# Zeroing the experts' sums on another engine, a new order of the first units' splits, and stores spread between loads

## Chip, cores and metric

The kernel runs on one core of one Trainium2 chip. The metric is the device time of one execution in microseconds; lower is better.

## Reference

Three layers follow each other, all in fp32.

```
attention: state = f[t]*state + outer(k[t], v[t]);  y[t] = q[t] @ state       B=4, H=8, S=768, D=48
gelu layer: h = x @ w_in;  g = h * sigmoid(1.702*h);  x2 = g @ w_out           x: 3072 x 384, FF=2048
experts:    p = probs / (sum(probs) + 1e-9)
            out = sum over e of p[:, e] * (relu(x2 @ w1[e]) @ w2[e])           E=4, w1[e]: 384 x 1024
```

## The kernel before

Every fp32 matrix product is made of three passes with operands split into a high part (fp32r, a copy made by ACT) and a low part (raw minus high, a subtraction by POOL or DVE): high by high, high by low, low by high.

**First part** (to about 660 us). Tokens are taken in 8 halves of 384. While the attention of half n+1 runs, the gelu layer of half n runs beside it, in slots: `hidden` for block `slot`, `layer_out` for block `slot - 2`. The last half (`moe(n)` on each engine, L850 for POOL, 16 blocks, 18 slots) has no attention beside it, so the engines prepare the first data of the experts there: weights of groups 0 and 1 and the tokens.

**Second part, the experts.** The 4 experts with 4 groups of 256 hidden columns each give 16 groups. Tokens come in three pairs of 1024 (`pr`). A unit is one group on one pair; 48 units: units 0 to 31 go over pairs 0 and 1 (groups 0 and 1 on pair 0, then on pair 1, then groups 2 and 3, ...), units 32 to 47 take pair 2 through all groups, with the weights loaded a second time (weight loads 16 to 31). On PE unit u is `first_layer(u)`, 33 matmuls of 512 columns with sums of blocks in place of a fourth of the products, and `second_layer(u)`, 48 matmuls of 384. The program order is first layer of unit 0, then for each u the first layer of u and the second layer of u-1. So units 0 and 1 have their first layers back to back.

What each engine does for unit u:

- ACT: `copy_x(u, 0..2)` (L1098) copies the bank `sum_x` to SBUF after the 1st, 2nd and 3rd stage of the first layer; `relu(u, 0..3)` (L1092) makes h_h.
- DVE: `sum_of(u, 1..5)` (L1410) adds banks and copies; `h_low(u, 0..3)` (L1416) makes h_l; `accumulate(u-1, 0..7)` (L1426) adds the second layer's result times the share to `acc`, the experts' sums (24 tiles of 128 tokens x 384, 8 a pair).
- PE's `first_layer(u)` waits in its middle for `hl_ready`, all four `h_low` of unit u-1, and for `x_copied`, the copies of unit u. PE's `second_layer` waits for the accumulations, since y has three banks.

`acc` lies in memory that earlier steps use, so it is set to zero late: by DVE in its loop over units, for pair 0 in unit 0 (L1442), for pairs 1 and 2 in units 2 and 4 (L1447), 3072 elements per partition each, always between the sums and the `h_low` and `accumulate` of that unit.

Preparing weights w: SP loads `we_raw` (L553) and `w_raw` (L558, named w2_raw in the code); POOL makes four sums of blocks (`weight_sums`, L801 to L809), ACT the high parts (`w1_high` L1064, `w2_high` L1072), POOL the low parts (`w1_low` L816, `w2_low` L827). Each of SP's loads waits until the low parts of the weights before are made. Preparing half-pair i of the tokens: SP loads `x_raw` (L567, x2_raw in the code, 2 DMAs) when the low parts of half-pair i-1 are made; sums of blocks (DVE L1355 to L1362 for i = 0 to 2, POOL L834 to L841 for i = 3), three high parts (`x_high`, ACT L1084), three low parts (`x_low`, DVE L1368 or POOL L847). Unit 0 needs half-pairs 0 and 1, unit 2 needs half-pairs 2 and 3.

All engines run their programs in order, and SP issues the DMAs in order: one queue, in which a wait holds up all that follows. ACT holds a fixed place for each split:

```
if u == 0:
    w2_high(1)
    for part in range(len(X_PARTS)):
        x_high(3, part)
```

stands behind unit 0's `relu`s and ahead of unit 1's `copy_x`. SP stores pairs 0 and 1 with two DMAs of 1536 KB (L591) between weight loads 18 and 19, once unit 31 is accumulated; pair 2 goes out tile by tile at the end (L598).

## Time and profile before

| | |
|---|---|
| median of 3 runs | 1444.72 us (1442.06 to 1447.53) |
| the profiled execution, its own time | 1443.81 us |
| its span, first to last instruction | 1442.1 us |
| PE busy in the span | 1397.3 us (97%) |
| DVE, POOL, ACT busy | 909.0, 633.6, 568.0 us |
| DMA share of its 16 engines | 23.4% |

The span is what the profiler saw between the first and the last instruction of this one execution; the execution's own time has 1.7 us around it. "Busy" adds up instructions and says nothing of which wait sets the end. PE is busy nearly all the time, so what can be gained without removing matmuls is at most the time in which PE waits, or runs at the lower clock. The lines of the rows below read: start in us from the span's start, duration, engine, line of the kernel, operation, output and input with their shapes, and in brackets how long the engine had stood idle before and who ended it. "x3" are three instructions in a row, and the duration is then that of all of them.

### The profile page before, as it was taken

To read this page: it belongs to the slowest core of one execution; us is meant where nothing else is said; L and a number is where in the kernel's file an instruction comes from. 1 tells how busy PE (TensorE), PEld (TensorE's weight loads), DVE (VectorE), ACT (ScalarE), POOL (GpSimd) and SP (SyncE) were. 2 spreads that over 40 slices of the span, in tenths; PEclk is the share of its full clock that TensorE was granted. 3 is DMA by queue.
4 is the path that set the end of the run, shared out by engine and by line. 5 is a ranking of instruction groups with operands and counts; after the bars stand their busy time and mean duration, and the time that the engine had idled before them with its cause. 6 is when DMAs were issued, how large, how long until landed. Compare 5 with 4: busy or idle time off the path is not lost.

```text
span 1442.1 us, 20967 instructions
## 1 busy us (share of the span) xinstructions
PE 1397.3 (97%) x8092; PEld 1315.9 (91%) x8092; DVE 909.0 (63%) x1375; ACT 568.0 (39%) x975; POOL 633.6 (44%) x711
## 2 busy tenths in 40 slices
PE   6889999999999999998999999999999999999999
PEld 5789999999999999996889999999999998999998
DVE  7785747565566656355666666666666666666666
ACT  5563534344444435244232233233223433343331
POOL 8785656556564737356122121222212363444430
PEclk9999999999999999999999999999999999999999
DMA  8534242332425150022010110101010113111111
GB/s 141 116 103 72 63 61 75 46 90 37 100 28 108 18 108 14 26 69 93 11 34 12 34 33 11 34 22 34 11 34 29 60 33 132 54 56 45 44 56 45
DMA packets 239700, 79.00 MB, mean 55 GB/s; under 512 B 188656, under 2 KB 238064, under 8 KB 239600
## 3 DMA queue, kind: packets, MB, share of 16 engines
q1 hardware_dynamic: 239600, 77.66, 23.4%
q8 instruction: 64, 1.05, 0.3%
q14 instruction: 36, 0.29, 0.1%
HBM read 67.83 MB, written 9.78 MB: 54 GB/s over the span
## 4 chain that ended last, share of the span: by engine, by line
PE 84%; POOL 5%; DVE 3%; ACT 3%; issue 2%; DMA 2%; SPq 0%; ACTq 0%; DVEq 0%; POOLq 0%
PE bank L1730 9%; PE bank L1732 9%; PE bank L1731 9%; PE bank L1679 8%; PE bank L1680 8%; PE bank L1681 8%; PE bank L1551 5%; PE bank L1643 4%; PE bank L1644 4%; PE bank L1645 4%; PE bank L1479 4%; PE bank L1477 4%; PE bank L1478 4%; PE bank L1590 2%; POOL g_l L779 2%
## 5 line engine op out<-in xcount | busy, mean ns | idle before, releaser
L1426 DVE SCALAR_TENSOR_TENSOR acc<-bank,p_n,acc 128x384 f32<-128x384 f32 x384 | 235.0, 613 | 67.5 <-PE bank L1732 63.0
L779 POOL TENSOR_TENSOR g_l<-sig,g_h 128x384 fp32r<-128x384 f32 x128 | 169.9, 1328 | 235.6 <-ACT g_h L1000 235.6
L1730 PE MATMUL bank<-w_h,h_h 128*128 128x384 f32 x768 | 258.2, 336 | 3.7 <-DVE acc L1426 3.7
L1732 PE MATMUL bank<-w_h,h_l 128*128 128x384 f32 x768 | 257.8, 336 | 0.0
L1731 PE MATMUL bank<-w_l,h_h 128*128 128x384 f32 x768 | 257.6, 335 | 0.0
L1410 DVE TENSOR_TENSOR bank<-bank,x_copy 128x512 f32<-128x512 f32 x192 | 124.6, 695 | 170.5 <-ACT x_copy L1098 106.0
L1679 PE MATMUL bank<-xs,we_h 128*128 128x512 f32 x528 | 207.0, 392 | 7.6 <-DVE h_l L1416 4.3
L1680 PE MATMUL bank<-xs,we_h 128*128 128x512 f32 x528 | 207.4, 393 | 0.0
L1681 PE MATMUL bank<-xs,we_l 128*128 128x512 f32 x528 | 207.3, 393 | 0.0
L816 POOL TENSOR_TENSOR we_l<-we_raw,we_h 128x384 fp32r<-128x384 f32 x96 | 97.0, 1039 | 237.3 <-ACT we_h L1064 237.3
L1322 DVE TENSOR_TENSOR sig<-bank,sig 128x384 f32<-128x384 f32 x128 | 71.0, 555 | 194.4 <-ACT sig L993 193.1
L1098 ACT ACTIVATE x_copy<-bank 128x512 f32<-128x512 f32 x144 | 86.2, 599 | 226.4 <-PE bank L1681 226.2
L1416 DVE SCALAR_TENSOR_TENSOR h_l<-bank,h_h 128x512 fp32r<-128x512 f32 x192 | 131.0, 683 | 31.9 <-ACT h_h L1092 31.9
L1730 PEld LDWEIGHTS bank<-w_h,h_h 128*128 128x128 f32 x768 | 144.6, 188 | 6.5 <-DVE acc L1426 4.3
L1092 ACT ACTIVATE h_h<-bank 128x512 fp32r<-128x512 f32 x192 | 114.9, 599 | 82.6 <-DVE bank L1410 82.6
L827 POOL TENSOR_TENSOR w_l<-w_raw,w_h 128x384 fp32r<-128x384 f32 x64 | 64.4, 1027 | 187.0 <-ACT w_h L1072 187.0
L1731 PEld LDWEIGHTS bank<-w_l,h_h 128*128 128x128 f32 x768 | 144.7, 188 | 1.9
L1732 PEld LDWEIGHTS bank<-w_h,h_l 128*128 128x128 f32 x768 | 144.6, 188 | 0.0
L1643 PE MATMUL bank<-g_h,wout_h 128*128 128x384 f32 x384 | 136.7, 356 | 3.0 <-POOL g_l L779 2.8
L1477 PE MATMUL bank<-x_h,win_h 128*128 128x384 f32 x384 | 128.4, 334 | 1.6 <-DVE x_l L1316 1.3
L1645 PE MATMUL bank<-g_h,wout_l 128*128 128x384 f32 x384 | 128.8, 335 | 0.0
L1644 PE MATMUL bank<-g_l,wout_h 128*128 128x384 f32 x384 | 128.7, 335 | 0.0
(145 smaller groups left out, 2565.7 us busy)
## 6 DMA issues: line engine op xcount, KB each, us to landing
we_raw<-in_moe_w SPq DMA_DIRECT2D x32, 384.0 KB, 3.9
w_raw<-in_moe_w SPq DMA_DIRECT2D x32, 384.0 KB, 3.2
v_sb<-in_v SPq DMA_DIRECT2D x24, 192.0 KB, 3.6
x_dram<-work SPq DMA_DIRECT2D x8, 576.0 KB, 3.2
x_raw<-x_dram SPq DMA_DIRECT2D x12, 384.0 KB, 4.0
f_raw<-in_f_logit SPq DMA_DIRECT2D x56, 72.0 KB, 2.2
q_raw<-in_q SPq DMA_DIRECT2D x56, 72.0 KB, 2.1
k_raw<-in_k SPq DMA_DIRECT2D x56, 72.0 KB, 2.1
```

Source lines behind the costliest of these rows:

```text
L779: pool.tensor_tensor(g_l[:, j % RING, :], sig[:, j % 2, :], g_h[:, j % RING, :].bitcast(F32), ALU.subtract).then_inc(gl_ready, 1)
L1426: dve.scalar_tensor_tensor(acc[:, pr * TT + i, :], y_bank[y % 3][:, 0:DM], p_n[:, col:col + 1], acc[:, pr * TT + i, :], ALU.mult, ALU.add) ...
L1477: pe.matmul(dst, lh, rh, start=i == 0, stop=False)
L1643: pe.matmul(dst, wh, gh, start=j == 0, stop=False)
L1644: pe.matmul(dst, wh, gl, start=False, stop=False)
L1645: last = pe.matmul(dst, wl, gh, start=False, stop=j == FT - 1)
L1679: pe.matmul(dst[:, :], lh, rh, start=start, stop=False, skip_group_check=True)
L1680: pe.matmul(dst[:, :], lh, rl, start=False, stop=False, skip_group_check=True)
L1681: return pe.matmul(dst[:, :], ll, rh, start=False, stop=True, skip_group_check=True)
L1730: pe.matmul(dst, hh, wh, start=f == 0, stop=False)
L1731: pe.matmul(dst, hh, wl, start=False, stop=False)
L1732: last = pe.matmul(dst, hl, wh, start=False, stop=f == 1)
```

## The change

Three things.

1. `acc` is set to zero by POOL instead of DVE, in 12 pieces of 768 elements (`clear`): pair 0 after the last half's `w1_low(1)`, pairs 1 and 2 after `w2_low(1)`. DVE waits for 4, 8 and 12 pieces where it waited for 1, 2 and 3 instructions.
2. The splits for the first units stand in another order. In the last half: `w1_high(0)` in slot 4 instead of 8 and `w2_high(0)` in slot 8 instead of 9 on ACT, with `w1_low(0)` and `w2_low(0)` four slots earlier on POOL and `weight_sums(1)` in slots 11 and 12 instead of 14 and 15; `x_high(0)`, `x_low(0)`, `x_sums(1)` one slot later. After the last slot: `w1_high(1)` ahead of `x_high(2, 0)`; DVE's third `x_low(2)` goes into unit 0, after its second sum. ACT's `w2_high(1)` and the three `x_high(3)` go from unit 0 into unit 1, the latter between its copies. POOL makes `x_sums(3)`, `x_low(3)` before `w2_low(1)`.
3. The two stores of 1536 KB become 8 of 384 KB, one behind each of the weight loads 19 to 26.

```diff
--- before.py
+++ after.py
@@ -585,19 +585,18 @@
             load_x(5)
             load_weights(GROUPS + 1)
             load_weights(GROUPS + 2)
-            for pr in range(2):
-
-                sp.wait_ge(acc_ready, (FIRST_THIRD - 2 + 2 * pr) * TT if pr == 0 else FIRST_THIRD * TT)
-                sp.dma_start(out_v[:, pr * TT:(pr + 1) * TT, :], acc[:, pr * TT:(pr + 1) * TT, :])\
-                    .then_inc(out_stored, 16)
+            sp.wait_ge(acc_ready, FIRST_THIRD * TT)
             for w in range(GROUPS + 3, W_LOADS):
                 load_weights(w)
+                lo = (w - GROUPS - 3) * 2
+                if lo < 2 * TT:
+                    sp.dma_start(out_v[:, lo:lo + 2, :], acc[:, lo:lo + 2, :]).then_inc(out_stored, 16)
             for i in range(TT):
 
                 sp.wait_ge(acc_ready, (UX - 1) * TT + i + 1)
                 sp.dma_start(out_v[:, 2 * TT + i, :], acc[:, 2 * TT + i, :]).then_inc(out_stored, 16)
 
-            sp.wait_ge(out_stored, 16 * (2 + TT))
+            sp.wait_ge(out_stored, 16 * (TT + TT))
 
 
         @block.gpsimd
@@ -791,6 +790,17 @@
                     for i in slot_pieces(n, slot):
                         weight_piece(i)
 
+            def clear(pr):
+                if pr == 0:
+
+                    pool.wait_ge(g_used, HALVES * FT)
+                else:
+
+                    pool.wait_ge(x2_stored, 16 * (HALVES + 1))
+                for i in range(pr * TT, (pr + 1) * TT, 2):
+                    last = pool.memset(acc[:, i:i + 2, :], 0.0)
+                    last.then_inc(acc_zero, 1)
+
             def weight_sums(w, part=None):
                 at_block = [we_raw[:, i * P:(i + 1) * P] for i in range(W_BLOCKS + 1)]
                 a21, a11, a22, a12 = at_block[0:4]
@@ -853,19 +863,22 @@
                         gelu_low(n, slot - 1)
                     if slot in (2, 3):
                         weight_sums(0, slot - 2)
-                    if 9 <= slot < 9 + W1_PARTS:
-                        w1_low(0, slot - 9)
-                    if 12 <= slot < 12 + W2_PARTS:
-                        w2_low(0, slot - 12)
-                    if slot in (14, 15):
-                        weight_sums(1, slot - 14)
+                    if 5 <= slot < 5 + W1_PARTS:
+                        w1_low(0, slot - 5)
+                    if 8 <= slot < 8 + W2_PARTS:
+                        w2_low(0, slot - 8)
+                    if slot in (11, 12):
+                        weight_sums(1, slot - 11)
                 w1_low(1)
+                clear(0)
 
             halves_program(alone, both, moe)
 
-            w2_low(1)
             x_sums(3)
             x_low(3)
+            w2_low(1)
+            clear(1)
+            clear(2)
             for u in range(UX):
                 for w in range(2, W_LOADS):
                     if last_unit[w - 2] + 2 == u:
@@ -1041,18 +1054,17 @@
                         gelu_sigmoid(n, slot)
                     if 1 <= slot <= FT:
                         gelu_high(n, slot - 1)
-                    if slot in (4, 5, 6):
-                        x_high(0, slot - 4)
+                    if slot in (5, 6, 7):
+                        x_high(0, slot - 5)
+                    if slot == 4:
+                        w1_high(0)
                     if slot == 8:
-                        w1_high(0)
-                    if slot == 9:
                         w2_high(0)
                     if slot in (10, 11, 12):
                         x_high(1, slot - 10)
-                x_high(2, 0)
                 w1_high(1)
-                x_high(2, 1)
-                x_high(2, 2)
+                for part in range(len(X_PARTS)):
+                    x_high(2, part)
                 read_x2(n)
 
             def w1_high(w):
@@ -1103,14 +1115,18 @@
                         w2_high(w)
                 copy_x(u, 0)
                 relu(u, 0)
+                if u == 1:
+                    x_high(3, 0)
                 copy_x(u, 1)
+                if u == 1:
+                    x_high(3, 1)
                 copy_x(u, 2)
+                if u == 1:
+                    x_high(3, 2)
                 for i in range(1, 4):
                     relu(u, i)
-                if u == 0:
+                if u == 1:
                     w2_high(1)
-                    for part in range(len(X_PARTS)):
-                        x_high(3, part)
                 for w in range(2, W_LOADS):
                     if last_unit[w - 2] == u:
                         w1_high(w)
@@ -1387,15 +1403,15 @@
                     gelu_product(n, slot)
                     if slot == 3:
                         x_sums(0)
-                    if slot in (5, 6, 7):
-                        x_low(0, slot - 5)
-                    if slot == 9:
+                    if slot in (6, 7, 8):
+                        x_low(0, slot - 6)
+                    if slot == 10:
                         x_sums(1)
                     if slot in (11, 12, 13):
                         x_low(1, slot - 11)
                 x_sums(2)
-                for part in range(len(X_PARTS)):
-                    x_low(2, part)
+                x_low(2, 0)
+                x_low(2, 1)
 
             halves_program(alone, both, moe)
 
@@ -1431,23 +1447,16 @@
                 sum_of(u, 1, sum_a[:, :], sum_a, 0)
                 h_low(u, 0)
                 sum_of(u, 2, x_copy[:, 1, :], sum_e, 1)
+                if u == 0:
+                    x_low(2, 2)
                 sum_of(u, 3, sum_c[:, :], sum_c, 2)
 
                 dve.wait_ge(sum_ready, 5 * u + 2)
                 sum_of(u, 4, sum_b[:, :], sum_b, 1)
                 sum_of(u, 5, sum_e[:, :], sum_e, 2)
-                if u == 0:
-
-                    dve.wait_ge(g_used, HALVES * FT)
-                    dve.memset(acc[:, 0:TT, :], 0.0).then_inc(acc_zero, 1)
-                if u in (2, 4):
-                    pr = u // 2
-
-                    dve.wait_ge(x2_stored, 16 * (HALVES + 1))
-                    dve.memset(acc[:, pr * TT:(pr + 1) * TT, :], 0.0).then_inc(acc_zero, 1)
                 if u in (1, 3, FIRST_THIRD + 1):
 
-                    dve.wait_ge(acc_zero, 1 + [1, 3, FIRST_THIRD + 1].index(u))
+                    dve.wait_ge(acc_zero, TT // 2 * (1 + [1, 3, FIRST_THIRD + 1].index(u)))
                 for i in range(1, 4):
                     if u:
                         accumulate(u - 1, i - 1)
```

Places in the order. **DVE**, from the last half's third set of tokens (L1355 to L1368) through unit 0 (L1410 are its sums, L1416 its h_l). Before:

```order
L1368 TENSOR_TENSOR xs_96<-x_raw,xs_96 128x3x256 [waits x2h_ready] x3
L1410 TENSOR_TENSOR bank<-bank,x_copy 128x512 [waits x_copied,ff_ready,p_step]
L1416 SCALAR_TENSOR_TENSOR h_l<-bank,h_h 128x512 [waits hh_ready]
L1410 TENSOR_TENSOR x_copy<-bank,x_copy 128x512 [waits x_copied,ff_ready]
L1410 TENSOR_TENSOR bank<-bank,x_copy 128x512 [waits x_copied,ff_ready]
L1410 TENSOR_TENSOR bank<-bank,x_copy 128x512 [waits ff_ready,sum_ready]
L1410 TENSOR_TENSOR bank<-bank,x_copy 128x512 [waits ff_ready]
L1442 MEMSET acc 128x3072 [waits g_used]
L1416 SCALAR_TENSOR_TENSOR h_l<-bank,h_h 128x512 [waits hh_ready] x3
```

and now (lines are shifted by 16: L1384 is `x_low`, L1426 `sum_of`, L1432 `h_low`):

```order
L1384 TENSOR_TENSOR xs_96<-x_raw,xs_96 128x3x256 [waits x2h_ready] x2
L1426 TENSOR_TENSOR bank<-bank,x_copy 128x512 [waits x_copied,ff_ready,p_step]
L1432 SCALAR_TENSOR_TENSOR h_l<-bank,h_h 128x512 [waits hh_ready]
L1426 TENSOR_TENSOR x_copy<-bank,x_copy 128x512 [waits x_copied,ff_ready]
L1384 TENSOR_TENSOR xs_96<-x_raw,xs_96 128x3x256 [waits x2h_ready]
L1426 TENSOR_TENSOR bank<-bank,x_copy 128x512 [waits x_copied,ff_ready]
L1426 TENSOR_TENSOR bank<-bank,x_copy 128x512 [waits ff_ready,sum_ready]
L1426 TENSOR_TENSOR bank<-bank,x_copy 128x512 [waits ff_ready]
L1432 SCALAR_TENSOR_TENSOR h_l<-bank,h_h 128x512 [waits hh_ready] x3
```

One `x_low` has moved behind the second sum, and the zeroing of 128x3072 in front of the three `h_low` is gone.

**ACT**, from unit 0's second copy on (L1098 copies, L1092 relus, L1072 is w2_high, L1084 x_high). Before:

```order
L1098 ACTIVATE x_copy<-bank 128x512 [waits ff_ready] x2
L1092 ACTIVATE h_h<-bank 128x512 [waits sum_ready] x3
L1072 ACTIVATE w_h_99<-w_raw 128x768 [waits w2_loaded]
L1084 ACTIVATE xs_96<-x_raw 128x3x256 [waits x2_loaded]
L1084 ACTIVATE xs_96<-x_raw 128x3x256 [waits x2_sums,x2_loaded] x2
L1098 ACTIVATE x_copy<-bank 128x512 [waits ff_ready]
L1092 ACTIVATE h_h<-bank 128x512 [waits sum_ready]
L1098 ACTIVATE x_copy<-bank 128x512 [waits ff_ready] x2
L1092 ACTIVATE h_h<-bank 128x512 [waits sum_ready] x3
```

and now (L1110 copies, L1104 relus, L1084 w2_high, L1096 x_high):

```order
L1110 ACTIVATE x_copy<-bank 128x512 [waits ff_ready] x2
L1104 ACTIVATE h_h<-bank 128x512 [waits sum_ready] x3
L1110 ACTIVATE x_copy<-bank 128x512 [waits ff_ready]
L1104 ACTIVATE h_h<-bank 128x512 [waits sum_ready]
L1096 ACTIVATE xs_96<-x_raw 128x3x256 [waits x2_loaded]
L1110 ACTIVATE x_copy<-bank 128x512 [waits ff_ready]
L1096 ACTIVATE xs_96<-x_raw 128x3x256 [waits x2_sums,x2_loaded]
L1110 ACTIVATE x_copy<-bank 128x512 [waits ff_ready]
L1096 ACTIVATE xs_96<-x_raw 128x3x256 [waits x2_sums,x2_loaded]
L1104 ACTIVATE h_h<-bank 128x512 [waits sum_ready] x3
L1084 ACTIVATE w_h_99<-w_raw 128x768 [waits w2_loaded]
```

Unit 1's first copy and relu stand directly behind unit 0's relus; each `x_high(3)`, with its wait for a load and for sums, now stands in front of a copy of unit 1 or of its relus.

**SP**, from weight load 18's second DMA on. Before:

```order
L558 DMA w_raw<-in_moe_w 128x2x384 [waits w2l_ready]
L591 DMA out_dram<-acc 128x8x384 [waits acc_ready] x2
L553 DMA we_raw<-in_moe_w 128x3x256 [waits w1l_ready]
L558 DMA w_raw<-in_moe_w 128x2x384 [waits w2l_ready]
L553 DMA we_raw<-in_moe_w 128x3x256 [waits w1l_ready]
L558 DMA w_raw<-in_moe_w 128x2x384 [waits w2l_ready]
L553 DMA we_raw<-in_moe_w 128x3x256 [waits w1l_ready]
```

and now:

```order
L558 DMA w_raw<-in_moe_w 128x2x384 [waits w2l_ready]
L553 DMA we_raw<-in_moe_w 128x3x256 [waits w1l_ready,acc_ready]
L558 DMA w_raw<-in_moe_w 128x2x384 [waits w2l_ready]
L593 DMA out_dram<-acc 128x2x384
L553 DMA we_raw<-in_moe_w 128x3x256 [waits w1l_ready]
L558 DMA w_raw<-in_moe_w 128x2x384 [waits w2l_ready]
L593 DMA out_dram<-acc 128x2x384
L553 DMA we_raw<-in_moe_w 128x3x256 [waits w1l_ready]
```

Weight load 19 no longer stands behind the two stores, and each piece of a store stands between two weight loads.

## Rows read from the trace of the kernel before

**Rows 1.** Waits of PE, whole run: releaser, us in total, times, longest.
```profile
PE bank L1730 <- DVE acc L1426: 3.7, 2, 1.8
...
PE bank L1679 <- ACT x_copy L1098: 3.4, 3, 1.8
```

**Rows 2.** Timeline of PE: start us, us, engine, line, operation, [idle before <-releaser].
```profile
659.74 0.39 PE L1679 MATMUL bank<-xs,we_h 128*128 128x512 f32 x1
...
666.27 0.50 PE L1679 MATMUL bank<-xs,we_h 128*128 128x512 f32 x1 [0.89 <-ACT x_copy L1098]
...
674.91 0.67 PE L1679 MATMUL bank<-xs,we_h 128*128 128x512 f32 x1 [4.25 <-DVE h_l L1416]
...
692.53 0.39 PE L1679 MATMUL bank<-xs,we_h 128*128 128x512 f32 x1
...
712.11 0.39 PE L1679 MATMUL bank<-xs,we_h 128*128 128x512 f32 x1
...
719.63 0.33 PE L1730 MATMUL bank<-w_h,h_h 128*128 128x384 f32 x1
...
727.97 0.39 PE L1679 MATMUL bank<-xs,we_h 128*128 128x512 f32 x1
...
746.23 0.39 PE L1679 MATMUL bank<-xs,we_h 128*128 128x512 f32 x1
...
1206.36 0.39 PE L1679 MATMUL bank<-xs,we_h 128*128 128x512 f32 x1
...
1224.39 0.39 PE L1679 MATMUL bank<-xs,we_h 128*128 128x512 f32 x1
```

**Rows 3.** Windows, PE: stretch, us, PE busy (matmuls), granted clock, DMA share, GB/s.
```profile
675.00:680.00 5.00, 4.37 (x10) 0.51 0.19 69
707.00:709.00 2.00, 2.00 (x8) 0.50 0.60 197
741.00:743.00 2.00, 2.00 (x13) 1.00 0.00 0
```

**Rows 4.** Timeline of DVE.
```profile
623.55 0.95 DVE L1368 TENSOR_TENSOR xs<-x_raw,xs 128x768 fp32r<-128x768 f32 x1
...
657.05 1.22 DVE L1355 TENSOR_TENSOR x_raw<-x_raw 128x256 f32<-128x256 f32 x1 [1.89 <-DMA x_raw<-x_dram]
...
659.33 5.17 DVE L1368 TENSOR_TENSOR xs<-x_raw,xs 128x768 fp32r<-128x768 f32 x3
...
673.03 1.82 DVE L1416 SCALAR_TENSOR_TENSOR h_l<-bank,h_h 128x512 fp32r<-128x512 f32 x3
...
702.11 2.62 DVE L1447 MEMSET acc<- 128x3072 f32 x1 [0.63 <-issue]
...
715.09 0.70 DVE L1410 TENSOR_TENSOR bank<-bank,x_copy 128x512 f32<-128x512 f32 x1 [2.16 <-ACT x_copy L1098]
...
719.17 1.90 DVE L1410 TENSOR_TENSOR bank<-bank,x_copy 128x512 f32<-128x512 f32 x3 [1.35 <-PE bank L1681]
```

**Rows 5.** Timeline of ACT, unit 3.
```profile
719.90 1.79 ACT L1092 ACTIVATE h_h<-bank 128x512 fp32r<-128x512 f32 x3 [0.84 <-DVE bank L1410]
```

**Rows 6.** Groups of POOL by form, and its timeline.
```profile
L680 POOL MEMSET state<- 128x384 f32 x4 | 1.7, 424 | 0.0
...
673.22 0.73 POOL L834 TENSOR_TENSOR x_raw<-x_raw 128x256 f32<-128x256 f32 x1
...
676.09 5.39 POOL L847 TENSOR_TENSOR xs<-x_raw,xs 128x768 fp32r<-128x768 f32 x3
```

**Rows 7.** Timeline of SP: the two loads of x_raw, third half.
```profile
652.01 1.00 SPq L567 DMA_DIRECT2D x_raw<-x_dram  x2
```

**Rows 8.** SP and POOL at the stores; the page's part on DMA issues.
```profile
1195.24 3.77 SPq L553 DMA_DIRECT2D we_raw<-in_moe_w  x1
...
1207.48 0.46 POOL L801 TENSOR_TENSOR we_raw<-we_raw 128x128 f32<-128x128 f32 x1 [13.82 <-DMA we_raw<-in_moe_w]
...
we_raw<-in_moe_w SPq DMA_DIRECT2D x32, 384.0 KB, 3.9
```

## Prediction

> **What bounds the kernel now.** I read the page's busy times first: PE works 1397.3 of 1442.1 us, and the change removes no matmul. So I asked for PE's waits, to see who ends them. Behind 659 us, where the experts begin, there are only six waits worth naming: one of 4.25 us for `h_low` (L1416) [rows 2], two of 1.8 us for accumulations (L1426), and three for `copy_x` (L1098), the longest 1.8, together 3.4 us [rows 1]. Then I read PE's timeline at the starts of the first layers, which prices each wait with all that it drags along [rows 2]. The reader is to see a steady beat and four places that miss it.
>
> The beat: from 746.23 (unit 5) to 1206.36 (unit 34) are 29 units, 15.87 us each. A first layer takes 719.63 - 712.11 = 7.52 us, a second 727.97 - 719.63 = 8.34 us. Against that:
>
> - A, units 0 and 1: 692.53 - 659.74 = 32.79 us for two first layers and one second, which at the beat are 23.38: **9.41 lost**.
> - B, unit 2 to 3: 712.11 - 692.53 = 19.58: **3.71 lost**.
> - C, unit 4 to 5: 746.23 - 727.97 = 18.26: **2.39 lost**.
> - D, unit 34 to 35: 1224.39 - 1206.36 = 18.03: **2.16 lost**.
>
> Together 17.67 us; nothing behind 660 us can give more. B and C have the same cause, the memset of 2.62 us on DVE [rows 4] ahead of the accumulation that frees a bank, and the same wait of 1.8 us. They differ by 1.32 us, and the windows say why: behind B's wait PE was granted 0.50 of the clock (1.2 instead of 2.4 GHz), behind C's all of it [rows 3]. Behind A's long wait it was 0.51 for the 5 us of the window, which is worth up to 2.5 us. A short wait thus costs its length, and sometimes 1.3 us more.
>
> **The change, part by part.** Times are counted from T = 659.74, unit 0's first matmul. T stays: the last half of the gelu layer has its splits in other slots, and a slot on POOL holds one g_l and at most one more subtraction, as before. One grain: POOL no longer has sums between the last two g_l, perhaps 0.2 us for PE; I leave it out.
>
> *B and C, the zeroing on POOL.* Both memsets leave DVE: 3.71 + 2.39 = **6.1 us gained**. Who waits now? DVE's first accumulation (about T+18) wants four pieces. A POOL memset of 384 elements takes 424 ns [rows 6]; a piece of 768 is then 0.42 (if size costs nothing) to 0.85 us (in proportion), I take 0.85, as nothing shows the fixed part here; four are 3.4. They start when POOL's `w1_low(1)` is done, which PE wants for unit 1 in any case, so at T+7.5 at the latest, and end by T+10.9: 7 us early. Pairs 1 and 2 are cleared at about T+22 to T+29, and are wanted at T+49 and in unit 33. Behind them on POOL stand `weight_sums(2)`, 2 us, done by T+31, for a copy that ACT wants when unit 2's relus end (unit 2's start + 9.6 us, T+34). Hidden, with 3 us in hand, and ACT itself has some 6 us after that until the next copy.
>
> *A, the first transition.* Now: DVE gets the third half-pair at 657.05, 5.0 us after its load was issued [rows 7, 4], makes three `x_low` in 5.17 us, does its first sum 1.7 us later than in unit 3, which makes `copy_x` and PE 0.89 us late [rows 2]; then the memset, then three `h_low` in 1.82 us from 673.03 [rows 4], on whose end PE resumes at 674.91. In the new order only two `x_low` precede unit 0, and their load is issued some 2 us earlier, since it no longer stands behind `w2_low(0)`. They end near T+1.5 to T+2.5; the first sum is due at T+3.0 (715.09 - 712.11 in unit 3 [rows 4]). The third `x_low` fits between the second sum's end, T+5.7, and the third's due time, T+7.06 (719.17 - 712.11), if it takes 0.95 us, as at 623.55, and not a third of 5.17, 1.72, as beside POOL's subtractions; beside it POOL now zeroes. Ends: 0 and 0.37 us late. I take 0.
>
> The Trainium skill (SBUF — State Buffer, "Who interferes with whom") says that a VectorE instruction with two SBUF inputs contends with a GpSimd instruction that reads SBUF, not with one that only writes it. The trace agrees for the first half (0.95 alone, 1.72 beside subtractions [rows 4]); no row has an `x_low` beside a memset. By the rule this term is 0, without it 0.37.
>
> Then nothing stands between unit 0's sums and its `h_low`: they start 1.8 us after the third sum, at T+8.86, and end 1.82 later; the relus end at 9.58 of a unit's time (719.90 + 1.79 - 712.11 [rows 5]) and do not hold them up. PE resumes at T+10.74. Its own work would bring it there at 7.52 + 9 matmuls of 0.228 = T+9.57. So a wait of 1.17 us stays, with 0.11 for the restart: A falls from 9.41 to 1.28, **8.1 us gained**. The clock may fall behind it: 0 (as behind C's wait and the 0.89 one) to 1.3 (as behind B's); I take 0, the shorter wait.
>
> *What ACT meets in unit 1.* `x_high(3, 0)` waits for a load that is issued later than before, at T+6.7, when the third `x_low` is done; with 5.0 us [rows 7, 4] it is there at T+11.7. ACT comes to it when unit 1's first relu ends, about T+12.0. POOL's four sums take 676.09 - 673.22 = 2.9 us [rows 6], to T+14.6, so `x_high(3, 1)` ends at T+15.5 and `copy_x(1, 2)` 0.3 us late, which PE doesn't see, as it needs only the copy before. POOL's three `x_low(3)` at 1.8 us [rows 6] end at T+20; unit 2 needs them at 10.74 + 24 x 0.228 + 8.34 = T+24.6. Cost 0, with under 0.5 us in hand at the load.
>
> *D, the stores.* Weight load 19 was issued at 1195.24 behind 3 MB of stores, and POOL had it 12.2 us later, where such a load lands in 3.9 [rows 8]: 8.3 us late, of which 2.16 reached PE, so some 6 us are in hand in each unit. Now load 19 goes ahead of all stores: **2.16 gained**. From load 20 on each `we_raw` stands behind 384 KB of store. Its price: 3 MB + 384 KB took 12.2, so a piece is some 1.1 to 1.4 us, with 0.5 for the issue under 2, against 6 in hand: 0.
>
> **Sum**: 6.1 + 8.1 + 2.16 = 16.4 us. The profiled execution took 1443.81 (span 1442.1, 1.7 around it), so 1427.4; the median of the runs is 0.9 above that execution, so I forecast **1428.3 us**, 1.1% less. Its own range is 1425 to 1431.
>
> **Rivals.** About 0.5% (7.2 us) is what a measurement of this kernel can tell from no change: the three runs are 5.5 us apart.
>
> 1. *The load of the fourth half-pair comes late.* It is now issued after work of unit 0, and ACT waits for it in front of two copies on which PE hangs. Each us beyond T+12.2 is a us for PE. Against it: 5.0 us is measured for the same two DMAs; for it: 0.5 us in hand, a weight load issued at its heels, and a store of 576 KB shortly ahead. At 7 us instead of 5, 2 us and a clock fall of up to 2.5 as in 675 to 680 [rows 3]: 1428.3 + 4.5 = **1432.8**. Chance 0.18. With 4 us of waits more, repeated for the sums, it leaves only B, C and D: 1444.72 - 8.3 = **1436.5**, chance 0.04.
> 2. *The stores do not come apart.* The pieces stand in the same queue, and if the load behind a piece is as late as that behind the whole, D stays, once: 1428.3 + 2.2 = **1430.5**. Chance 0.05.
> 3. *Slower: the pieces hit eight times.* The mechanism is D's, at weight loads 20 to 27: late `we_raw`, ACT holding `w1_high` in front of `copy_x`. It decides when a piece makes its load more than 6 us late; to be slower than before by over 7.2 us each must cost PE (14.2 + 2.2 + 7.2)/8 = 3 us, a lateness of 9 us, or a piece as bad as 3 MB was. Then 1444.7 + 7.4 = **1452**. For it speaks only that eight units are touched where one was. Chance 0.02.
> 4. *Nothing measurable*: POOL's queue turns late. If a piece takes more than about 1.6 us (twice my value) the clears push `weight_sums(2)` beyond ACT's last moment; at 2.5 us a piece, 20 us more on POOL and some 10 for PE: **1438 to 1441**. Chance 0.03. The Trainium skill (GPSIMD Engine Reference, "4.1 Engine selection") advises VectorE over GpSimd for elementwise work, about 2x slower with two inputs, near line rate with one; the memset rows agree with the last (424 ns for 384 elements on POOL, 2618 for 3072 on DVE, 1.1 and 0.85 ns each).
>
> **Numbers.** My forecast has 0.68. Rivals 1 and 2 are still over 0.5% faster: with the forecast 0.94, rounded down for half of rival 4. Faster 0.93, same 0.05, slower 0.02. The range: 1424 (forecast's low end less 1 for another day's median) to 1436 (rivals 1 and 2 inside).
>
> **What would show it.** In the new trace: no L1442 or L1447 on DVE and twelve POOL memsets near 0.7 to 0.85 us; first layers from unit 2 on 15.87 us apart without exception; PE waiting 1.0 to 1.2 us for `h_low` near T+9.6 and for nothing else until the end; unit 2 starting near T+24.6; POOL taking weight load 19 under 5 us after its issue. Wrong it would be if PE waits for `copy_x` in unit 1 (rival 1), for `copy_x` in units 35 to 43 (2, 3), for accumulations or w1_low in units 2 to 4 (4), or if the last half's slots before T get longer.

## Result, and the profile after

| | before | after |
|---|---|---|
| median | 1445.55 us (4 runs, 1442.06 to 1447.53) | 1428.82 us (4 runs, 1426.74 to 1435.15) |
| profiled execution, its own time | 1443.81 us | 1427.06 us |
| its span | 1442.1 us | 1425.3 us |
| PE busy | 1397.3 us | 1390.6 us |

The changed kernel takes 0.9894 of the time of the kernel before, 95% interval 0.9855 to 0.9933: 1.1% faster. 1428.3 us was forecast, within 1424 to 1436.

The page's first lines of the changed kernel:

```profile
span 1425.3 us, 20983 instructions
...
PE 1390.6 (98%) x8092; PEld 1312.1 (92%) x8092; DVE 906.2 (64%) x1372; ACT 568.6 (40%) x975; POOL 634.6 (45%) x723
```

PE's waits from 657 us to the end (releaser, us in total, times, longest), to be held against [rows 1]:

```profile
PE bank L1688 <- DVE h_l L1432: 1.1, 1, 1.1
PE bank L1688 <- ACT x_copy L1110: 0.2, 1, 0.2
```

Of the six waits behind 659 us two are left, 1.3 us together. The timeline of PE at T (unit 0's first matmul), at the wait, and at unit 2's first matmul, against [rows 2]:

```profile
658.79 0.39 PE L1688 MATMUL bank<-xs,we_h 128*128 128x512 f32 x1
...
670.09 0.50 PE L1688 MATMUL bank<-xs,we_h 128*128 128x512 f32 x1 [1.07 <-DVE h_l L1432]
...
684.01 0.39 PE L1688 MATMUL bank<-xs,we_h 128*128 128x512 f32 x1
```

T is now 658.79 and unit 2 starts at 684.01, 25.22 us later, where it was 32.79. All later first layers start 15.87 us apart, with no exception, up to the last at 1398.03. So the span's 16.8 us come out as T 0.95, A 7.57, B 3.71, C 2.39, D 2.16: together 16.78.

DVE around unit 0 (lines are 16 higher than in [rows 4]):

```profile
654.50 1.26 DVE L1371 TENSOR_TENSOR x_raw<-x_raw 128x256 f32<-128x256 f32 x1
...
659.16 2.64 DVE L1384 TENSOR_TENSOR xs<-x_raw,xs 128x768 fp32r<-128x768 f32 x2
662.66 0.70 DVE L1426 TENSOR_TENSOR bank<-bank,x_copy 128x512 f32<-128x512 f32 x1 [0.87 <-ACT x_copy L1110]
...
665.23 0.95 DVE L1384 TENSOR_TENSOR xs<-x_raw,xs 128x768 fp32r<-128x768 f32 x1
666.36 1.89 DVE L1426 TENSOR_TENSOR bank<-bank,x_copy 128x512 f32<-128x512 f32 x3 [0.18 <-PE bank L1690]
668.16 1.88 DVE L1432 SCALAR_TENSOR_TENSOR h_l<-bank,h_h 128x512 fp32r<-128x512 f32 x3
```

The reader is to see that no memset is left between the sums that start at 666.36 and the three `h_low` at 668.16, and that the third `x_low`, at 665.23, takes 0.95 us and fits ahead of the sums. The sums of blocks (from 654.50, four of 1.1 to 1.3 us, done at T+0.45) are slower than I had them; that holds back ACT's second `x_high(2)`, the next rows, and through it unit 0's first copy.

ACT, from the second `x_high(2)` on:

```profile
659.33 1.59 ACT L1096 ACTIVATE xs<-x_raw 128x768 fp32r<-128x768 f32 x2 [2.40 <-DVE x_raw L1378]
660.82 1.23 ACT L1021 ACTIVATE work<-bank 128x384 f32<-128x384 f32 x3
661.92 0.61 ACT L1110 ACTIVATE x_copy<-bank 128x512 f32<-128x512 f32 x1
...
671.17 0.83 ACT L1096 ACTIVATE xs<-x_raw 128x768 fp32r<-128x768 f32 x1
672.47 0.60 ACT L1110 ACTIVATE x_copy<-bank 128x512 f32<-128x512 f32 x1 [0.46 <-PE bank L1690]
```

POOL: pair 0's four memsets, the first sum for the fourth half-pair with the DMA that it waited for, and the eight memsets of pairs 1 and 2; and the group's line (us busy, mean ns):

```profile
660.05 2.79 POOL L801 MEMSET acc<- 128x768 f32 x4
670.73 0.74 POOL L844 TENSOR_TENSOR x_raw<-x_raw 128x256 f32<-128x256 f32 x1 [7.88 <-DMA x_raw<-x_dram]
...
680.98 5.51 POOL L801 MEMSET acc<- 128x768 f32 x8
```

```profile
L801 POOL MEMSET acc<- 128x768 f32 x12 | 8.3, 745 | 0.0
```

Stores: SP issues a piece and then weight load 20; POOL takes the load at 1200.63, against [rows 8]:

```profile
1195.36 0.47 SPq L593 DMA_DIRECT2D out_dram<-acc  x1
1195.87 0.47 SPq L553 DMA_DIRECT2D we_raw<-in_moe_w  x1
```

```profile
1200.63 0.46 POOL L811 TENSOR_TENSOR we_raw<-we_raw 128x128 f32<-128x128 f32 x1 [5.71 <-DMA we_raw<-in_moe_w]
```

The load is in POOL's hands 4.8 us after its issue; load 19, with no store ahead, took 3.9 in this trace and 12.2 before.

### The profile page after: what moved, and what is told of

It reads as the page before. It is cut to its first block, busy times and chain, and to the rows that moved or that the text cites. A ratio compares the mean times of both kernels' runs of the same rounds, so it can differ in the third digit from the quotient of the medians.

```text
span 1425.3 us, 20983 instructions
## 1 busy us (share of the span) xinstructions
PE 1390.6 (98%) x8092; PEld 1312.1 (92%) x8092; DVE 906.2 (64%) x1372; ACT 568.6 (40%) x975; POOL 634.6 (45%) x723
## 3 DMA queue, kind: packets, MB, share of 16 engines
q8 instruction: 64, 1.05, 0.3%
## 4 chain that ended last, share of the span: by engine, by line
PE 88%; POOL 4%; DVE 3%; ACT 2%; issue 2%; SPq 1%; DMA 0%; POOLq 0%; DVEq 0%; ACTq 0%
PE bank L1741 9%; PE bank L1739 9%; PE bank L1740 9%; PE bank L1689 8%; PE bank L1690 8%; PE bank L1688 8%; PE bank L1560 5%; PE bank L1652 4%; PE bank L1654 4%; PE bank L1653 4%; PE bank L1486 4%; PE bank L1488 4%; PE bank L1487 4%; PE bank L1599 3%; POOL k_T L714 1%
## 5 line engine op out<-in xcount | busy, mean ns | idle before, releaser
L778 POOL TENSOR_TENSOR g_l<-sig,g_h 128x384 fp32r<-128x384 f32 x128 | 161.8, 1265 | 241.1 <-ACT g_h L1013 241.1
L1426 DVE TENSOR_TENSOR bank<-bank,x_copy 128x512 f32<-128x512 f32 x192 | 124.6, 695 | 164.1 <-ACT x_copy L1110 100.7
L1110 ACT ACTIVATE x_copy<-bank 128x512 f32<-128x512 f32 x144 | 86.1, 598 | 221.5 <-PE bank L1690 221.3
L1432 DVE SCALAR_TENSOR_TENSOR h_l<-bank,h_h 128x512 fp32r<-128x512 f32 x192 | 130.9, 682 | 31.9 <-ACT h_h L1104 31.9
L1104 ACT ACTIVATE h_h<-bank 128x512 fp32r<-128x512 f32 x192 | 114.9, 599 | 80.1 <-DVE bank L1426 80.0
```

Source lines behind the costliest of these rows:

```text
L778: pool.tensor_tensor(g_l[:, j % RING, :], sig[:, j % 2, :], g_h[:, j % RING, :].bitcast(F32), ALU.subtract).then_inc(gl_ready, 1)
```

## Experiments

All were read by the same few numbers. T moves by several us from run to run while the first part of the program is the same or nearly so, so the stretches behind T tell more than times do.

| kernel | T | T to unit 2 | unit 2 to 3 | 4 to 5 | longest of 34 to 36 | span |
|---|---|---|---|---|---|---|
| before | 659.74 | 32.79 | 19.58 | 18.26 | 18.03 | 1442.1 |
| b_pool_zero | 663.44 | 33.36 | 15.87 | 15.87 | 17.72 | 1440.0 |
| b_new_order | 661.71 | 31.26 | 19.56 | 18.23 | 17.95 | 1442.4 |
| b_new_stores | 659.96 | 31.54 | 18.24 | 18.24 | 15.87 | 1437.5 |
| changed | 658.79 | 25.22 | 15.87 | 15.87 | 15.87 | 1425.3 |
| a_old_stores | 662.45 | 24.71 | 15.87 | 15.87 | 17.91 | 1430.5 |
| a_act_old | 661.86 | 31.21 | 15.87 | 15.87 | 15.87 | 1434.4 |
| a_slots_old | 659.42 | 25.96 | 15.87 | 15.87 | 15.87 | 1426.7 |
| a_two_stores_apart | 659.58 | 25.21 | 15.87 | 15.87 | 15.87 | 1426.1 |
| a_both_behind_19 | 661.52 | 25.22 | 15.87 | 15.87 | 17.08 | 1429.3 |
| a_clear_x4 | 659.21 | 25.60 | 15.87 | 15.87 | 15.87 | 1426.1 |
| a_late_third_low | 658.62 | 29.39 | 15.87 | 15.87 | 15.87 | 1429.3 |
| a_sum_c_first | 661.13 | 25.03 | 15.87 | 15.87 | 15.87 | 1427.5 |
| a_best | 662.34 | 24.52 | 15.87 | 15.87 | 15.87 | 1428.2 |

The beat alone would be 23.38 in the third column.

Not all of that column is the code's. The ten kernels with the new slots run the same work up to T, and yet are of two kinds. In five (changed, b_new_order, a_two_stores_apart, a_both_behind_19, a_sum_c_first) DVE's first sum of blocks takes 1.1 to 1.3 us, the four sums end at T+0.45, and PE pauses 0.2 us for unit 0's first copy, near T+3.8. In the other five (a_old_stores, a_act_old, a_clear_x4, a_late_third_low, a_best) that sum starts 0.3 us earlier and takes 0.42, the four end at T-0.7, and there is no pause. In a_old_stores, where T is 662.45, the first two sums and unit 0's copy are:

```profile
657.89 0.42 DVE L1372 TENSOR_TENSOR x_raw<-x_raw 128x256 f32<-128x256 f32 x1
658.22 1.22 DVE L1373 TENSOR_TENSOR x_raw<-x_raw 128x256 f32<-128x256 f32 x1
...
664.73 0.60 ACT L1111 ACTIVATE x_copy<-bank 128x512 f32<-128x512 f32 x1
```

The copy starts at T+2.28 there and at T+3.13 in the changed kernel's trace, and all that follows is 0.5 us earlier. Up to the stores a_old_stores is the changed kernel, and so are a_two_stores_apart and a_both_behind_19 (25.21, 25.22): the changed kernel's third column is 24.71 or 25.22, by the execution. Kernels of the second kind are therefore held against 24.71. The kernel before varies too: b_new_stores is the same code up to unit 31, and has 31.54 instead of 32.79. Its pause for the copy was 0.55 us instead of 0.89, and the clock was at the lower level from T+13.0 to T+19.8 instead of T+15.3 to T+22.2, so that more of this fell into the wait for `h_low`.

### The parts alone: the zeroing (b_pool_zero)

```diff
 # before, POOL
+    clear(0)              # behind w1_low(1) of the last half
 ...
+    clear(1); clear(2)    # behind x_low(3)
 # before, DVE
-    dve.memset(acc[:, 0:TT, :], 0.0)                 # unit 0
-    dve.memset(acc[:, pr * TT:(pr + 1) * TT, :], 0.0)  # units 2 and 4
```

> The kernel before with only the zeroing moved to POOL in twelve pieces. Theory (each wait is priced by itself): B and C vanish, so units 2 to 3 and 4 to 5 start 15.87 us apart (6.1 us gained); in A the wait for h_low shrinks by the memset and its issue, 3.25 us, from 4.25 to about 1.0, and with it goes most of the slow-clock stretch, so A loses 9.41 - 3.3 - 1 to 2.5 = 3.6 to 5.1; D stays at 2.2. Span about 1442 - 6.1 - 5 = 1431, gain 10.4 to 11.9 us. Rival (a new wait takes the place of the memset, since ACT still makes w2_high(1) and x_high(3) ahead of unit 1's copies): A stays above 6.5 us and the gain is under 9.

Measured: 1438.73 us median of 6 runs, 0.995 of before (0.9928 to 0.9971). B and C are gone to the last hundredth and D stayed (1.85 us), but A did not shrink: 33.36 us, my theory's 27 to 28.5 was wrong and the rival right. PE's two waits in unit 1:

```profile
675.41 0.50 PE L1684 MATMUL bank<-xs,we_h 128*128 128x512 f32 x1 [1.05 <-DVE h_l L1430]
...
682.03 0.79 PE L1684 MATMUL bank<-xs,we_h 128*128 128x512 f32 x1 [4.97 <-ACT x_copy L1112]
```

The wait for `h_low` fell from 4.25 to 1.05 us, as reckoned, and a wait of 4.97 for `copy_x` stands behind it in place of 0.63. ACT shows why (w2_high, the first x_high(3), the other two, unit 1's copy):

```profile
674.09 0.83 ACT L1086 ACTIVATE w_h<-w_raw 128x768 fp32r<-128x768 f32 x1
674.83 0.83 ACT L1098 ACTIVATE xs<-x_raw 128x768 fp32r<-128x768 f32 x1
679.92 1.58 ACT L1098 ACTIVATE xs<-x_raw 128x768 fp32r<-128x768 f32 x2 [4.26 <-POOL x_raw L852]
681.40 0.58 ACT L1112 ACTIVATE x_copy<-bank 128x512 f32<-128x512 f32 x1
```

ACT stood 4.26 us at `x_high(3, 1)` for POOL's sums, with unit 1's copy behind it. Before, this ran under the memset: PE's restart behind the copy is at T+18.6 in both (678.34 - 659.74 and 682.03 - 663.44). As long as ACT makes `x_high(3)` there, the memset in unit 0 costs nothing. The third column is 0.6 us larger than before, for the lower clock lasted to T+23.3 instead of T+22.2.

### The order alone (b_new_order)

The second part of the diff on all engines, zeroing and stores as before.

> The kernel before with only the new order of the splits (zeroing on DVE, two stores of 1536 KB as before). Theory: B, C and D stay (8.3 us, of which up to 1.3 is the clock's chance); in A the wait for copy_x of 0.89 us goes but the memset stays between the sums and h_low, so PE waits 1.1 + 3.25 = 4.3 us for h_low as before; A loses 9.41 - 0.5 to 1.6 = 7.8 to 8.9. Gain 1 to 2 us, within noise of the runs. Rival (the order is the main part): A falls under 5 us, gain over 4.

Measured: 1441.91 us, 10 runs, 0.9979 of before (0.9962 to 0.9996). A is 31.26, 1.5 us less; the memset holds the wait for `h_low` at its old size:

```profile
PE bank L1684 <- DVE h_l L1419: 4.3, 1, 4.3
PE bank L1735 <- DVE acc L1429: 3.7, 2, 1.8
```

That is what was expected (7.9 us lost), but most of the 1.5 can be the execution's: b_new_stores, the kernel before's own code up to unit 31, is 1.25 us shorter too. Ahead of the clock's part, PE's restart behind the wait for `h_low` is at T+14.50, against T+15.17 before and T+14.82 in b_new_stores: the order alone is worth 0.3 to 0.7 us.

So of A's 7.57 us the zeroing alone gives -0.6 and the order alone 1.5, with the clock's chance in both, and together they give 7.6: 6.6 us belong to neither, only to the pair (7.9 with b_new_stores' 31.54 as the start).

### Which part of the order (a_act_old, a_slots_old)

```diff
 # changed kernel, ACT, a_act_old
 copy_x(u, 0); relu(u, 0)
-if u == 1: x_high(3, 0)
 copy_x(u, 1)
-if u == 1: x_high(3, 1)
 copy_x(u, 2)
-if u == 1: x_high(3, 2)
 for i in range(1, 4): relu(u, i)
-if u == 1: w2_high(1)
+if u == 0: w2_high(1); x_high(3, 0); x_high(3, 1); x_high(3, 2)
```

> The changed kernel, but ACT makes w2_high(1) and the three x_high(3) in unit 0 again, ahead of unit 1's first copy; everything else of the new order stays. Theory (from the run with the zeroing alone: ACT's place for x_high(3) was a second cause hidden behind the memset): the wait for h_low is 1.1 us as now, but copy_x(1, 0) stands behind sums that POOL ends near T+15 and two copies of 0.8 us, so PE waits some 5 us for it and then runs at the lower clock; T to unit 2 goes from 25.2 to 30.5 to 33. Rival (the order of DVE and of the last half was what mattered): T to unit 2 under 27.

Measured: T to unit 2 31.21. `x_high(3)` from its first on, unit 1's copy, and PE:

```profile
672.97 0.85 ACT L1096 ACTIVATE xs<-x_raw 128x768 fp32r<-128x768 f32 x1 [0.79 <-DMA x_raw<-x_dram]
676.03 1.58 ACT L1096 ACTIVATE xs<-x_raw 128x768 fp32r<-128x768 f32 x2 [2.21 <-POOL x_raw L851]
677.51 0.58 ACT L1110 ACTIVATE x_copy<-bank 128x512 f32<-128x512 f32 x1
```

```profile
678.14 0.79 PE L1684 MATMUL bank<-xs,we_h 128*128 128x512 f32 x1 [3.83 <-ACT x_copy L1110]
```

The copy starts at 677.51, 1.48 us behind `x_high(3, 1)`, which waited for POOL. PE waits 3.83 us, then runs at the lower clock (granted 0.55 from 676 to 680). ACT's move is worth 6.5 us of A once the memset is away, 31.21 against 24.71.

a_slots_old puts the splits of the last half back in their slots (POOL 9, 12, 14; ACT 4 to 6, 8, 9; DVE 5 to 7 and 9), the rest as changed.

> The changed kernel with the splits of the last half back in their old slots; what stands behind the last slot keeps the new order. Theory: this part is small: the last half's stretch from its first wait for g_l to T is 0.4 us longer (46.8 instead of 46.4), the third half-pair is loaded 2 us later, and T to unit 2 grows from 25.2 by 0 to 1 us. Rival (the earlier load is what carries the transition): T to unit 2 over 27.

Measured: T to unit 2 25.96, 0.74 more than 25.22 and 1.25 more than 24.71. DVE's first sum of blocks comes later:

```profile
656.66 1.29 DVE L1371 TENSOR_TENSOR x_raw<-x_raw 128x256 f32<-128x256 f32 x1 [1.82 <-DMA x_raw<-x_dram]
```

656.66 is T-2.8, where the changed kernel has 654.50, T-4.3. PE waits 0.94 us for unit 0's first copy; before the change it was 0.89 us, for the second. The stretch from the last half's first wait for g_l to T is 46.73 us here and 46.18 in the changed kernel; over the kernels with the old slots it is 46.66 to 46.97 (four), over those with the new 46.18 to 46.72 (ten). The means are 0.3 us apart, and the place is the end: from PE's last wait of 0.5 us or more for g_l to T are 3.60 to 3.89 us with the old slots and 3.24 to 3.26 with the new. So 0.3 us of T's 0.95 are the change's; the rest lies ahead of the last half, in code that is the same.

What DVE's place for the third `x_low(2)` and POOL's `x_sums(3)` ahead of `w2_low(1)` give was not undone by itself; how they share in the rest of the order's gain is not shown.

### The stores (a_old_stores, b_new_stores, a_both_behind_19, a_two_stores_apart)

Two undo and redo the third part of the diff alone.

> The changed kernel with the two stores of 1536 KB back between weight loads 18 and 19. Theory: only D returns: unit 34 to 35 takes 18.0 us instead of 15.87 with a wait of 1.8 us for copy_x, POOL has weight load 19 about 12 us after its issue; span 2.2 us longer than the changed kernel's, about 1427.5. Rival (D was the first part's or chance): no unit of the second part is longer than 15.9 us.

Measured: D is back, 17.91 instead of 15.87, with a wait of 1.75 us for `copy_x`; D costs 2.04. (Its span is 5.2 us longer: 3.7 of that is T, 2.0 is D, and A is 0.5 shorter, as it is of the second kind.)

> The kernel before with only the stores in eight pieces. Theory: A, B, C as before (9.4, 2.4 to 3.7, 2.4 to 3.7), D gone; units 31 to 47 all 15.87 us apart; POOL has the weight loads behind a piece 5.5 to 6 us after the store's issue. It also shows B and C once more: if the clock's fall behind a wait of 1.8 us is a matter of chance, B and C may swap their 3.7 and 2.4. Span about 1440. Rival (pieces hit several times): waits for copy_x in units 35 to 43.

Measured: D gone, no wait in the third part, A to C still there. B and C are both 18.24 here. The windows behind their waits of 1.84 us (stretch, us, PE busy, granted clock, DMA share, GB/s):

```profile
704.00:706.00 2.00, 1.82 (x10) 1.00 0.00 0
738.00:740.00 2.00, 1.72 (x9) 1.00 0.00 0
```

Full clock both times, unlike B in [rows 3].

The other two ask whether size or place decides:

```diff
 # a_both_behind_19
-    if lo < 2 * TT: sp.dma_start(out_v[:, lo:lo + 2, :], ...)
+    if w == GROUPS + 3: two stores of 1536 KB
 # a_two_stores_apart
+    w == GROUPS + 3: one store of 1536 KB;  w == GROUPS + 4: the other
```

> The changed kernel with both stores of 1536 KB behind weight load 19, ahead of 20. Theory (size against what a unit hides decides, not the place): load 20 is 8 to 9 us late and PE waits 1.5 to 2.5 us for copy_x in unit 35; span about 2 us longer. Rival (load 18 to 19 was a special place, as the wait for unit 31's accumulation stands there): no wait, all units 15.87.

Measured: weight load 20, issued at 1199.24, in POOL's hands and PE's wait:

```profile
1210.57 0.47 POOL L811 TENSOR_TENSOR we_raw<-we_raw 128x128 f32<-128x128 f32 x1 [12.90 <-DMA we_raw<-in_moe_w]
```

```profile
1214.88 0.50 PE L1688 MATMUL bank<-xs,we_h 128*128 128x512 f32 x1 [0.91 <-ACT x_copy L1110]
```

A unit of 17.08, 1.21 lost, less than my 2 but of the kind. Against the usual 3.9 us the load was 7.4 late; before, 8.3 late cost 2.16. Both give the same border: 7.4 - 1.2 = 6.2 and 8.3 - 2.2 = 6.1 us that a unit hides.

> The changed kernel with two stores of 1536 KB again, one behind weight load 19 and one behind 20. By the lateness that a unit can hide (some 6 us, since 8.3 us late cost 2.2) a store of 1.5 MB, which makes the load behind it some 4 to 5 us late, costs nothing: no unit of the third part above 15.9 us, POOL has the weight 9 to 10 us after the store's issue. Rival (any big store ahead of a load reaches PE): one or two units of 16.5 us or more with waits for copy_x.

Measured: no wait at all. The loads, issued at 1196.69 and 1213.31, were taken 7.6 and 7.7 us later:

```profile
1204.32 0.46 POOL L811 TENSOR_TENSOR we_raw<-we_raw 128x128 f32<-128x128 f32 x1 [8.58 <-DMA we_raw<-in_moe_w]
...
1221.03 0.46 POOL L811 TENSOR_TENSOR we_raw<-we_raw 128x128 f32<-128x128 f32 x1 [8.68 <-DMA we_raw<-in_moe_w]
```

3.7 us late, under the border. Two stores instead of eight would have done; what counts is that no more than some 6 us of transfer stand ahead of one load.

### Memsets beside DVE (a_clear_x4)

```diff
 # changed kernel, POOL, clear(0)
+    for again in range(4):   # each round waits for the one before
         4 memsets of 768 elements
```

> The changed kernel, but pair 0 is zeroed four times over on POOL, 16 memsets or some 11.5 us instead of 2.8, so that memsets now lie beside DVE's third x_low(2). By the rule that a GpSimd instruction which only writes SBUF doesn't contend, that x_low keeps its 0.95 us, sums and h_low start as before, and PE's wait for h_low stays 1.1 us; T to unit 2 stays 25.2 us, up to 0.6 more if POOL's sums for the fourth half-pair start a little late. Rival (memsets contend too): the x_low takes 1.3 to 1.8 us and PE's wait grows by 0.3 or more. It also shows whether twelve memsets more on POOL cost PE anything; theory: under 0.6 us.

Measured: POOL's 16 memsets, and DVE's `x_low(2)`, the first two together and then the third:

```profile
661.01 11.32 POOL L804 MEMSET acc<- 128x768 f32 x16
```

```profile
658.42 3.47 DVE L1387 TENSOR_TENSOR xs<-x_raw,xs 128x768 fp32r<-128x768 f32 x2
...
664.84 0.95 DVE L1387 TENSOR_TENSOR xs<-x_raw,xs 128x768 fp32r<-128x768 f32 x1
```

The third `x_low`, at 664.84, lies wholly beside memsets and takes 0.95 us; the first two began beside POOL's subtractions and took 3.47. That is the rule that the prediction weighed (the Trainium skill, SBUF — State Buffer, "Who interferes with whom"), and here the trace bears it out. In the changed kernel the clears end at 662.84, ahead of the third `x_low`, but the second one there already lay beside them, and the two took 2.64 us, not 3.47.

Twelve memsets more cost PE 0.9 us, not under 0.6. The third column, 25.60, has no pause at the first copy and so stands against 24.71; against 25.22 the price would seem 0.38. The sums behind the memsets on POOL start at T+13.1 instead of T+11.1 (a_old_stores), ACT's second `x_high(3)` and a copy of unit 1 behind it are late, so are DVE's sums and its first accumulation, and PE waits:

```profile
679.24 0.44 PE L1742 MATMUL bank<-w_h,h_h 128*128 128x384 f32 x1 [0.33 <-DVE acc L1445]
```

### The margin at the fourth half-pair (a_late_third_low)

```diff
 # changed kernel, DVE, unit 0
 sum_of(u, 2, ...)
-if u == 0: x_low(2, 2)
 sum_of(u, 3, ...); sum_of(u, 4, ...); sum_of(u, 5, ...)
+if u == 0: h_low(u, 1..3); x_low(2, 2)
```

> The changed kernel with DVE's third x_low(2) behind unit 0's h_low instead of behind its second sum, so that the load of the fourth half-pair is issued about 5 us later (T+12 instead of T+7.4). Theory (my rival 1, a margin of 0.5 us): ACT stands at x_high(3, 0) until T+17, copy_x(1, 1) is 3 to 4 us late for PE, and T to unit 2 grows from 25.2 to 28.5 to 30, with up to 2 us on top if the clock falls. PE's wait for h_low stays 1.1 us or shrinks by 0.3. Rival (there is slack behind that load): T to unit 2 stays under 26.

Measured: T to unit 2 29.39. ACT's `x_high(3, 0)` with its wait for the DMA, and the copy behind it; then PE's window behind its wait (granted clock 0.60):

```profile
674.69 0.84 ACT L1096 ACTIVATE xs<-x_raw 128x768 fp32r<-128x768 f32 x1 [3.23 <-DMA x_raw<-x_dram]
675.44 0.58 ACT L1110 ACTIVATE x_copy<-bank 128x512 f32<-128x512 f32 x1
```

```profile
676.00:680.00 4.00, 3.93 (x11) 0.60 0.00 0
```

The load was issued at 670.25 instead of 666.20, 4.2 us later counted from T; PE waited 2.92 us and lost 4.7 in all, 29.39 against 24.71. The wait for `h_low` was 1.07, as in all kernels without the memset and with PE's old order (1.05 to 1.07). Moving this one subtraction behind unit 0's own work costs over a quarter of the gain: the mechanism of rival 1 is there, and the changed kernel stays 0.4 us clear of it (load at 670.73, ACT there at 671.17; 0.75 us in a_old_stores).

### A shorter transition (a_sum_c_first, a_best)

```diff
 # changed kernel, PE, first_layer, unit 1
+if u == 1: pe.wait_ge(hl_ready, 4 * (u - 1) + 2); both products of sum_c
 pe.wait_ge(hl_ready, 4 * u)
 sum_e, sum_b
 # a_best, ACT, besides
-x_high(2, 2)               # ahead of read_x2
+x_high(2, 2)               # behind copy_x(0, 0)
```

> The changed kernel, but unit 1's first layer makes the two products of bank sum_c (6 matmuls, 1.4 us) ahead of the wait for all four h_low of unit 0; they need only the second. Theory: the wait for h_low near T+9.8 is cut from 1.1 us to under 0.5, and T to unit 2 from 25.2 to about 24.2. Rival (the wait moves to ACT's copies of unit 1): T to unit 2 stays at 25.0 or more, with waits for copy_x.

Measured: 25.03, and the rival is right. The wait for `h_low` is gone, but a wait of 0.69 for `copy_x(1, 1)` came: those 6 matmuls had been what covered this copy.

> As a_sum_c_first, and on ACT the third x_high(2) goes behind unit 0's first copy, so that this copy is no longer 0.85 us late. Theory: the pause of 0.34 us near T+3.5 goes, the third sum starts at T+7.1 instead of T+7.6, and T to unit 2 is 23.5 to 24.0 (the beat alone is 23.4). Against the kernel before: 17 to 18 us less, 1.2 to 1.3%; against the changed kernel 1.3 us less, which the times alone can't show. Rival: relu(0, 0) behind the moved x_high is late and T to unit 2 stays above 24.2.

Measured: 24.52, not under 24.0. There is no pause near T+3.5, but four kernels without this edit have none either, so no run shows that the edit did it. Kind against kind, the early `sum_c` gives 0.2 us (25.03 against 25.22, 24.52 against 24.71) and the moved `x_high(2, 2)` nothing beyond. The wait for the copy stays:

```profile
676.35 0.50 PE L1690 MATMUL bank<-xs,we_h 128*128 128x512 f32 x1 [0.69 <-ACT x_copy L1110]
```

1426.78 us, median of 4 runs, 0.987 of before (0.9844 to 0.9895). Its stretch from T is 0.7 us shorter than the changed kernel's, 0.5 of it by the kind of execution; the intervals overlap, and as a time it can't be told from it.

## Why the prediction was right, and where a step was not

- **The inventory.** PE's lost time by first layers (9.41, 3.71, 2.39, 2.16) held, and so did "nothing behind 660 us can give more". It also made the sum robust: each part was read against the beat.
- **B and C, 6.1 us**: gained in full. A piece takes 745 ns, four 2.79 us, against my 0.85 us and 3.4. Nobody waited for POOL's clears, but the work behind them has little in hand: four times the clearing for pair 0 cost 0.9.
- **D, 2.16 us**: gained; pieces cost 0. "Some 6 us in hand" came as 6.1 us before and as 6.2 from another place and lateness (a_both_behind_19). A piece makes its load 0.9 us slower, with 0.5 for its issue: my 1.6 to 1.9 was a bit high.
- **A, 8.1 us**: 7.57 came. The wait for `h_low` was predicted as 1.17 + 0.11 for the restart and came as 1.46 and 0.34 us between matmuls where 0.23 is the pitch, so 1.34. The rest, 0.45, is PE's pause for unit 0's first copy, a term that my sum did not have. I had followed DVE alone, from its two `x_low` to its first sum "due at T+3.0". But that sum needs `copy_x(0, 0)`, and on ACT this copy stands behind `read_x2` and, ahead of that, `x_high(2, 1)` and `x_high(2, 2)`, which wait for DVE's four sums of blocks. Those took 4.7 us instead of 2.3, each beside one of POOL's subtractions, so the copy started at T+3.13 instead of T+2.28. (The two `x_low` ended at T+3.0, not at T+1.5 to T+2.5, but DVE then still waited 0.87 us for that copy.) In a_old_stores, the same code up to the stores, the first of those sums took 0.42 us, DVE's first sum started at T+3.0, and A gave 32.79 - 24.71 = 8.08, my number. Which of the two comes is decided where DVE's first sum and POOL's g_l start within 0.02 us of each other (0.16 in b_new_order); that an execution falls to either side by chance is inferred.
- **The clock**: my 0 held, in all kernels with a wait of 1.07 us only; my reason, "the shorter wait", is not shown. Behind 1.84 us the clock fell in two of six (B before, B in b_new_order), worth 1.3 us each, and not in b_new_stores; and in the first part it fell behind waits shorter than 1.07 (last section).
- **T**: some 0.3 us of gain that I had put at 0.2 and left out; the rest of its 0.95 is no part of the change, but of where this one execution stood in a spread of 4.8 us.
- **What the prediction did not say**: it let the reader think that the memset's departure was most of A. It was not; alone it gives nothing there (b_pool_zero). The right sum came out because the diff moved ACT's `x_high(3)` too, and I had followed ACT through unit 1. My own expectation for b_pool_zero shows the error that was near.

Summed: 6.1 + 7.57 + 2.16 + 0.95 = 16.8 against 16.4. The parts B, C and D are the mechanism's. That the whole comes within 0.4 us is in part luck: A's missing 0.5 and T's 0.95 partly cancel, and the four times of the changed kernel are 8.4 us apart.

## What to carry to other kernels

When two waits follow each other closely on the bottleneck engine, ask for each at what time the engine would restart if the other were gone; two causes that end at the same time are worth nothing one by one and all of it together. Price a late transfer by the lateness that the consumer hides (here 6 us a unit), found from one case in which it reached the bottleneck, and cut or spread what stands ahead of the load until it is under that. Work on an idle engine is free only if what is queued behind it there is wanted late.

## What the runs showed of the hardware that I had not expected

- DVE's sums of blocks, 256 elements with both inputs in SBUF, take 0.41 to 0.43 us alone and 1.1 to 1.3 beside POOL's subtractions of 384, three times as long; DVE's subtractions of 768 elements take 0.95 against 1.7 to 1.8. The short ones suffer most, as each seems to wait for a whole instruction of the other (inferred from the lengths, not tested by itself). Beside POOL's memsets there is no such effect (0.95, a_clear_x4).
- The same wait of 1.84 us lowered the granted clock to 0.50 in two of six cases and left it at 1.00 in four. The four waits of 1.56 to 1.83 us at D (before, b_new_order, b_pool_zero, a_old_stores) left it at 1.00 as well. Yet between 500 and 520 us of the changed kernel PE's longest wait is 0.67 us, ended at 510.39, and from 513 to 516 PE had 0.50 of the clock (stretch, us, PE busy, granted clock, DMA share, GB/s). Which waits lower it, no run here explains; their length alone does not decide.

```profile
513.00:516.00 3.00, 3.00 (x12) 0.50 0.58 72
```

- T lay between 658.62 and 663.44 in the 14 profiles, though the program up to 600 us is the same in all. T goes with the clock in those 600 us: T was 658.79 to 659.74 in the four traces with 3 to 7 us at the lower clock, 658.62 to 661.71 in the five with 10, and 661.52 to 663.44 in the five with 14 to 17. The whole times do the same: of the 24 executions of the kernel before that have one on record, the four with a mean granted clock of 0.996 took 1438.2 to 1440.8 us, the two with 0.989 took 1449.0 and 1449.7. So most of the spread of the times goes with the clock; what sets the clock's course was not tested.
